# Two MLPs behind block attention: the first MLP by seven products as well, its weights prepared by GpSimd while two small tiles run

## The reference

```python
scores = scale * np.matmul(q_c, k_c.transpose(0, 1, 2, 4, 3))    # chunks of 64 tokens, 8 batches, 8 heads of 64
attn = exp(scores - max); attn = attn / (sum + 1e-09); out = np.matmul(attn, v_c)

gate = 1.0 / (1.0 + np.exp(-(x @ w_gate)))                       # first MLP, 512 -> 1536 -> 512
x2 = (gate * (x @ w_val)) @ w_out

h = x2 @ w_in                                                    # second MLP, 512 -> 2048 -> 512
g = np.where(h >= 1, h, np.where(h <= -1, 0.0, (h + 1) ** 2 / 4))
y = g @ w_out
```

## Time and profile before

| | |
|---|---|
| median of 3 runs | 1730.79 us (1730.62 to 1734.08) |
| the profiled execution | 1734.57 us, of which the span is 1732.7 us |
| mean granted clock | 0.995 |
| busy: TensorE, VectorE, ScalarE, GpSimd | 1717.8, 839.3, 719.5, 312.4 us |
| DMA | 300.48 MB, mean 173 GB/s |
| GpSimd waiting for its next piece of weights | 388.8 us in 32 waits |
| ScalarE's table loads | 65, 1283 ns each |
| first MLP ends, second begins | 1030.3, 1031.7 us |

### The profile page before, as it was taken

The page is one execution under the profiler, slowest core; times in us unless marked ns, Lnnn a source line. Parts: engine busy times, 40 slices in busy tenths (PEclk is TensorE's granted clock), DMA queues, the critical chain, the costliest instruction groups (busy, mean ns, idle before and its releaser), DMA issues.

```text
span 1732.7 us, 24808 instructions
## 1 busy us (share of the span) xinstructions
PE 1717.8 (99%) x9216; PEld 1543.0 (89%) x9216; DVE 839.3 (48%) x1220; ACT 719.5 (42%) x1033; POOL 312.4 (18%) x654
## 2 busy tenths in 40 slices
PE   7999999999999999999999999999999999999999
PEld 6888888888888888888888889999999999999999
DVE  3432323323223233232332237958858679588585
ACT  2332323313323233232331137557556475575563
POOL 5741423504325144142300000000000000000000
PEclk8999999999999999999999999999999999999999
DMA  5432414424234143241411137778877788788775
GB/s 212 157 93 87 142 56 142 136 73 143 73 114 147 52 148 107 98 137 49 158 43 61 43 110 283 283 257 301 282 282 287 244 297 289 254 301 283 250 284 177
DMA packets 97937, 300.48 MB, mean 173 GB/s; under 512 B 9760, under 2 KB 53792, under 8 KB 80928
## 3 DMA queue, kind: packets, MB, share of 16 engines
q1 hardware_dynamic: 87456, 251.69, 41.8%
q10 hardware_dynamic: 10368, 47.19, 8.1%
HBM read 250.61 MB, written 48.23 MB: 172 GB/s over the span
## 4 chain that ended last, share of the span: by engine, by line
PE 99%; DMA 1%; ACTq 0%; ACT 0%; DVE 0%; issue 0%
PE banks L601 7%; PE banks L599 7%; PE banks L624 7%; PE banks L623 7%; PE banks L622 7%; PE banks L600 7%; PE gate_ps L512 6%; PE out_ps L543 6%; PE out_ps L545 6%; PE gate_ps L513 6%; PE gate_ps L514 6%; PE val_ps L513 6%; PE val_ps L514 6%; PE val_ps L512 6%; PE out_ps L544 6%; PE att_ps L505 3%
## 5 line engine op out<-in xcount | busy, mean ns | idle before, releaser
L1034 DVE TENSOR_TENSOR g_full<-val_ps,act_buf 128x512 f32<-128x512 f32 x108 | 74.7, 692 | 474.7 <-PE val_ps L514 446.0
L599 PE MATMUL banks<-combo_hi,ring 128*128 128x384 f32 x672 | 224.5, 334 | 1.2 <-ACT chain L830 1.2
L624 PE MATMUL banks<-split_hi,ring 128*128 128x384 f32 x672 | 224.5, 334 | 0.0
L622 PE MATMUL banks<-split_hi,ring 128*128 128x384 f32 x672 | 224.5, 334 | 0.0
L623 PE MATMUL banks<-split_lo,ring 128*128 128x384 f32 x672 | 224.5, 334 | 0.0
L601 PE MATMUL banks<-combo_hi,ring 128*128 128x384 f32 x672 | 224.5, 334 | 0.0
L600 PE MATMUL banks<-combo_lo,ring 128*128 128x384 f32 x672 | 224.5, 334 | 0.0
L783 ACT ACTIVATE g_hi<-g_full 128x512 fp32r<-128x512 f32 x108 | 68.2, 632 | 287.4 <-DVE g_full L1034 287.4
L512 PE MATMUL gate_ps<-x_hi,weights 128*128 128x512 f32 x432 | 175.8, 407 | 0.1
L543 PE MATMUL out_ps<-g_hi,weights 128*128 128x512 f32 x432 | 171.5, 397 | 0.0
L545 PE MATMUL out_ps<-g_hi,weights 128*128 128x512 f32 x432 | 168.7, 391 | 0.0
(11 more groups left out here) (112 smaller groups left out, 3031.1 us busy)
## 6 DMA issues: line engine op xcount, KB each, us to landing
ring<-w_out_split SPq DMA_DIRECT2D x84, 1024.0 KB, 5.7
ring<-w_in_split SPq DMA_DIRECT2D x48, 1024.0 KB, 5.2
ring<-w_in_split SPq DMA_DIRECT2D x48, 768.0 KB, 6.6
tile_in<-q_k_dram ACTq DMA_DIRECT2D x33, 768.0 KB, 4.7
tile_in<-v_dram ACTq DMA_DIRECT2D x33, 512.0 KB, 3.8
w_in_split<-stage SPq DMA_DIRECT2D x112, 128.0 KB, 1.7
w_out_split<-stage SPq DMA_DIRECT2D x112, 128.0 KB, 1.8
x_in<-x_scratch SPq DMA_DIRECT2D x6, 1536.0 KB, 8.8
```

Of the source, the lines that this page charges most:

```text
L599: pe.matmul(ps, w_lo, hi, start=first and k == 0, stop=False, skip_group_check=more)
L622: pe.matmul(ps[:, j, :], w_lo, hi, start=first and k == 0, stop=False, skip_group_check=more)
L624: last = pe.matmul(ps[:, j, :], w_hi, hi, start=False, stop=k == NU - 1, skip_group_check=more)
```

## The change

The first MLP is done in two ways now. Two tiles of 384 tokens (0 and 1) keep the old form with the resident weights, with matmuls of 384 columns. The other 3840 tokens go in five passes of 768 tokens by seven products, as the second MLP does: 12 units (gate and value in turn) of 7 x 6 matmuls, then 7 products of 3 pairs on the way out. Then come the six passes of the second MLP as before. Rounds of attention are 6 chunks long, 48 in all: 12 between the thirds of chunks in the two tiles and 8 in each of passes 0 to 3, one a unit (TensorE: scores after the unit's first product, the transposes before its last, `mix` ahead of the next unit).

GpSimd prepares 34 pieces now (18 for the first MLP, 16 for the second), with 256 columns an operation, and starts when the value products of tile 0 are done, since three of its buffers lie over that tile's low parts. The ring loads of pass 0 wait for what they read. SP issues in one order: 9 pieces around the first five ring loads, then three stored products after each ring load until the 18 pieces are done, then one.

The sigmoid is written as (1 + tanh(x/2))/2: ScalarE takes tanh, VectorE does (t + 1) * v in one operation, and the half is applied to the outputs. q, k and v come without zeros; VectorE writes the zeros once, with 16 memsets, and ScalarE's queue issues four loads a round.

```diff
+TILES = 2
+MLP1 = 5
+MLP2 = 6
+PASSES = MLP1 + MLP2
...
+            return bank((0, 2, 1)[u % 3] if second(p) else (6, 7)[u % 2])
...
+            def store_prepared(at):
+                piece, n = at // 7, at % 7
+                sp.wait_ge(prep_split, at + 1)
+                done = prep_stored[at % 3] if at < PIECES_1 * 7 else prep2_stored[at % 2]
+                place = prep_place(at).rearrange("p a l n -> p (a l n)")
+                sp.dma_start(place, prep_out(at)).then_inc(done, DMA)
+                if piece + 1 < PIECES:
+                    if n == 4:
+                        load_raw(piece + 1, 1)
+                    if n == 5:
+                        load_raw(piece + 1, 0)
+                    if n == 6:
+                        load_raw(piece + 1, 2)
+                        load_raw(piece + 1, 3)
...
+            def load_ring(p, n):
+                now = load_index(p, n)
+                if now < RING:
+                    sp.wait_ge(val_done, C1 + 7 + n)
+                else:
+                    used, count = freed(now - RING)
+                    sp.wait_ge(used, count)
+                if p == 0:
+                    at = 7 * (n // 2) + 6
+                    if n >= 2 * n_units(p):
+                        at = 7 * (PIECES_1 - 1) + PREP.index(order(p)[(n - 2 * n_units(p)) // 2])
+                    for b in range(3):
...
+            for u in range(3 * C1):
+                load_stage(u)
+            sp.wait_ge(w_split, 3 * C1)
+            for b in range(4):
+                load_raw(0, b)
+            prepared = 0
+            for upto, loads in ((6, (0,)), (7, (1,)), (8, (2, 3)), (9, (4,))):
+                while prepared < 7 * upto:
+                    store_prepared(prepared)
+                    prepared += 1
+                for n in loads:
+                    load_ring(0, n)
+
+            for p in range(PASSES):
+                for n in range(RING if p == 0 else 0, n_loads(p)):
+                    load_ring(p, n)
+                    for _ in range(3 if prepared < PIECES_1 * 7 else 1):
+                        if prepared < 7 * PIECES:
+                            store_prepared(prepared)
+                            prepared += 1
...
+            pool.wait_ge(val_done, C1)
             for piece in range(PIECES):
+                if piece == 12:
+                    pool.wait_ge(out_bank_done, TILES * KT)
+                if piece == PIECES_1:
+                    for b in range(2):
+                        pool.wait_ge(prep_stored[b], DMA * 7 * PIECES_1 // 3)
                 prepare(piece)
...
+            def output(p):
+
+                kps, final = n_pairs(p), n_units(p) - 1
+                if second(p):
+                    pe.wait_ge(g21_ready, tiles(p, 6))
+                elif p + 1 < MLP1:
+                    pe.wait_ge(x_saved, round_of(p + 1, 8) - 2 * NR)
+                else:
+                    pe.wait_ge(x_saved, round_of(p, 8) - 2 * NR)
...
+            for p in range(PASSES):
+                first_unit(p, 2 if p == 0 else 0)
+                for u in range(1, n_units(p)):
+                    attends = p + 1 < MLP1
+                    if attends and 2 <= u <= 9:
+                        mix(round_of(p + 1, u - 2))
+                    one, two, three, four, five = order(p)[0:5]
+                    unit(p, u, one)
+                    if attends and u <= 8:
+                        scores(round_of(p + 1, u - 1))
+                    unit(p, u, two)
+                    unit(p, u - 1, 4)
+                    unit(p, u, three)
+                    unit(p, u, four)
+                    unit(p, u - 1, 3)
+                    if attends and u <= 8:
+                        transpose_probs(round_of(p + 1, u - 1))
+                    unit(p, u, five)
+                output(p)
+            out_pair(PASSES - 1, 3, n_pairs(PASSES - 1) - 2)
...
-                act.activation(act_buf[:, :], gate_ps[:, :], ACT.Sigmoid).then_inc(gate_read, 1)
+                act.activation(act_buf[:, :], gate_ps, ACT.Tanh, scale=0.5).then_inc(gate_read, 1)
...
+            def tanh1(p, u):
+                act.wait_ge(h22_ready, units(p, u))
+                act.activation(hg[:, :, :], hg[:, :, :], ACT.Tanh, scale=0.5).then_inc(t1_ready, 1)
...
+            def gated1(p, m):
+                dve.wait_ge(h22_ready, units(p, 2 * m + 1))
+                dve.wait_ge(t1_ready, tiles(p, m))
                 if p and m == 0:
-                    dve.wait_ge(y_stored[0], DMA * p)
-                dve.tensor_tensor(h1[:, 0, :], y_bank(m), chain1[:, m % 2, :], op=ALU.add).then_inc(h11_ready, 1)
```

1759 lines of the change are left out of this document (969 added, 790 removed).

## The result

| | median us | runs | ratio to before |
|---|---|---|---|
| before | 1730.7 | 1730.05 to 1734.08 | 1 |
| after | 1821.4 | 1818.91 to 1827.32 | 1.0525 [1.0496, 1.0554] |

The forecast was 1714 (1670 to 1752). The time is 107 us above it and outside the range, on the other side of no change.

The account below looks back on a forecast made before the run. TensorE, 99% busy, was taken as the bound: 1659 us without waits, plus 40 stall, 12 sharing and 5 slips gave 1716 span, 1718 execution, and 1714 as median. The 8-in-10 range was 1670 to 1752.

Parts of the forecast that it names:

- TensorE's stream: First MLP and attention: narrower matmuls save 76.7 us, 48 shorter attention rounds add 8; a pass with attention takes 154.
- the 1659: Whole kernel: the span in us if TensorE never waited, 74 less than 1732.7.
- The prologue: Before the first MLP: smaller loads and fewer matmuls bring it from 36.9 us to 30, ends 28 and 35.
- The rate of GpSimd: Weight preparation for the first MLP: 13.2 us a piece in tile 1, 14.3 in pass 0.
- the stall: Pass 0: TensorE waits 40 us for late weights, reaching the way out at 357 us; ends 8 and 78.
- The term for transfers: GpSimd's pieces: 0.7 us wait for a raw block; pass 0 adds 1.1 for VectorE's heavier work and DMA engines.
- The demand of 430 GB/s: Pass 0: 4.3 MB moved in a 10 us unit, where the fullest window in the profile moved 419 GB/s.
- The end of 16 us a piece: Slow end for GpSimd's pace: the way out of pass 0 at 395 us, a stall of 78.
- a stall over 60: Sign for pass 0: a stall under 15 us or over 60 makes the GpSimd rate wrong.
- Sharing in the ways out: Passes 0 to 2: VectorE and GpSimd exclude each other, +4 us each way out, +12 in all.
- The clock: Rival: it falls in pass 0, +73 us, 1787; sign is under 1.0 after 60 us; chance 11%.
- Keeping up: Rival: GpSimd takes 12.2 us a piece, so the stall is about 13 and the time 1685; chance 17%.

Follow-up runs that it names:

- without preparation: Changed kernel with nothing prepared while it runs: ring loads take fixed blocks, GpSimd idles after its splits, no raw loads or stores; 1678.3 us, ratio 0.968.
- work alone: Changed kernel with GpSimd's full casts and subtractions but no raw loads or stores of results; ring loads take fixed blocks yet wait for their product; 1726.4 us, 0.9955.
- all mends: Changed kernel with earlier start, more buffers, second raw set, new product order, second MLP's pieces outside ways out, one wait less; 1738.9 us, 1.0028.
- moves alone: Changed kernel with all transfers and waits kept, but GpSimd's operations on weight pieces cut to 4 columns, except the first products; 1762.6 us, 1.016.

## Why the prediction was wrong, point by point

- **TensorE's stream was right in the passes.** Passes with attention take 153.9 us without preparation, 154 forecast, and the gate by tanh and the narrower matmuls cost what was worked out. Three sizes in the 1659 were off: without stalls TensorE reaches the way out of pass 0 at 324.5 us, not 315 to 318, of which 4 us are there when tile 0's values end (GpSimd's start at 119.0 for 115); pass 4 takes 136.3 for 131; and the second MLP takes 1.4 us more in each of five passes, because a wait that only its first pass needs was set for each. Together some 20 us: the kernel without preparation has a span of 1677.7, 19 above the 1659.
- **The prologue shrank less.** Tile 0's last value product, GpSimd's start, comes 4 us late. The windows answer to the earlier trace rows: where the DMA engines moved 414 GB/s before, they move 220 to 241 at a full share. v comes in runs of 256 bytes now, which may be the reason; no run changes that alone.

```profile
4.00:8.00 4.00, 0.53 (x6) 0.56 (x8) 3.31 (x10) 0.00 (x0) 3.55 (x4) 1.00 1.05 241
12.00:16.00 4.00, 1.55 (x12) 1.15 (x12) 1.57 (x6) 2.31 (x4) 1.88 (x2) 1.00 1.15 220
```

- **The rate of GpSimd is the step that failed.** "I take 14.3 us a piece" in pass 0; it was 18.2. By the prediction's terms the eighteenth piece was due at 364 us (115 + 8 x 13.2 + 10 x 14.3) and ended at 422.7, 59 late: 4 for the start, 4 in the first six pieces, 12 in the seventh and eighth, 39 in the last ten. TensorE reached the way out 59 us after the 357 of the forecast as well. So the stall was 91 us and not 40. The part that rested on operations held: 12.5 us with VectorE in tile 1 and at most 13.6 in pass 0, against 12.7 and 13.4 measured with work alone. The term for transfers failed: 0.7 us of raw wait and a share of 1.1, where the runs put 4.8 us a piece on it in pass 0 (18.2 less 13.4). I had read 2.0 us for a raw block off the stores of a queue that was idle around them, where now 1 MB loads and 256 KB stores stand ahead of it; and stores, three buffers deep, had no term.
- **The demand of 430 GB/s was set against the wrong time.** It was worked out for a unit of 10 us. By the prediction's own rate GpSimd paces a unit at 12.3 us, six products, which makes it 350; at 15.6 us a unit it is 276, and 287 GB/s were measured in 264 to 404 us at a share of 0.89. So the changed kernel never asked for the fullest window, and its transfers still took up to twice as long as assumed. The 430 is what a kernel would ask for that keeps up: the one with all mends moved 360 GB/s with the engines full, and its small transfers took 7 to 10 us.
- **The bound was too narrow.** The end of 16 us a piece (a stall of 78) was in the text, and the range went only to 1752. The stall alone came to more than that end, and by the prediction's own sign (a stall over 60) the rate was wrong.
- **Sharing in the ways out was right in kind and near in size.** The ways out of passes 1 and 2 are 5 and 6 us longer for the 4 forecast, shown with work alone (+6) and moves alone (0), and `split_lo` has a mean of 1211 ns there for 951. In pass 0 it was 18, where work alone gives 10 and moves alone 11: that is late pieces as much as sharing. Outside the way out passes 1 and 2 lost 9 us each, for which I gave nothing; moves alone show about all of it, work alone 1 to 2.
- **The rivals.** The clock did fall, to 0.61 and 0.84, and I had given it 1787. But matmuls that held it at 0.98 changed nothing, so that the time lies on that rival's side is no merit of it, and a clock under 1.0, which I had named as its sign, could not tell cause from consequence. Keeping up is excluded by work alone, 13.4 us a piece for the 12.2 of that rival. The rival that was missing: work and transfers are both slower than TensorE needs, and half of the transfers' time stands behind the work.

## What to carry to other kernels

When weights are prepared while they are needed, price the loop transfer, operation, store, buffer free as one chain, with transfer times of a loaded queue, and not the operations alone. Work out the demand for bandwidth over the time that your own sum gives the stretch. Where it then comes to the fullest window, take that as a bound of its own, and expect every other stream (here attention's v) to pay too. A clock that is harmless while another engine sets the pace can cost again when that is mended. An idle stretch of the engine that will set the pace is the first thing to use: 36 us of it gave 30 back.

## What the runs showed of the hardware

- A 128 KB load took 4.1 us (median) at a DMA share of 0.73 to 0.89 and 8.1 us at 1.02, on the same queue; a 256 KB store 3.5 to 4.9 and 6.4 to 9.6. The 1 MB loads took 7.4 to 8.0 and 7.1.
- GpSimd at 256 columns: cast 0.40 us undisturbed and 0.40 to 0.51 on average in 224 to 404 us, subtraction 0.73 and 0.75 to 0.80. On 4 columns of each block the same operations still took 0.20 to 0.31 us. In the ways out of passes 1 and 2 ScalarE's fourth to last split is 6 us longer while GpSimd works, and unchanged when only transfers run; VectorE's subtraction of 768 columns has a mean of 1211 to 1220 ns there for 951.
- With the DMA engines fully busy the prologue's loads came at 220 to 241 GB/s; in the kernel before, 414 to 419. Later in the changed kernel, from 224 to 404 us, 5.51 MB of attention's queue took 11.9% of the engines' time and 43.87 MB of SP's 73.2%: 2.16% and 1.67% a MB.
- Nothing read the 20 extra matmuls a unit, and they held the clock at 0.98 for 0.84 without changing the time. In the kernel with all mends the clock was 0.75 to 0.88 in the units in which TensorE waited or ran slowly, and 1.00 in those between.
